# Attention and two gated MLPs on one core: the first pairs' transposes, sums and quotients move between the three banks

## The reference

```python
def phi(x):                      # x = q or k, scaled by D ** -0.25
    h = einsum('bhsd,md->bhsm', x, omega) - sum(x * x, -1) / 2
    return exp(h - max(h, -1)) / sqrt(m)
kv  = einsum('bhsm,bhsd->bhmd', k_p, v)
z   = sum(k_p, axis=2)
num = einsum('bhsm,bhmd->bhsd', q_p, kv)
den = einsum('bhsm,bhm->bhs', q_p, z) + 1e-06
x   = num / den                  # heads side by side: 2304 x 512
h = x @ w_in;  x = (h * clip(h + 3, 0, 6) / 6) @ w_out
h = x @ w_in2; x = (h * sigmoid(1.702 * h)) @ w_out2
```

## Time and profile before

| | us |
|---|---|
| median of 3 runs | 951.43 |
| lowest, highest | 950.95, 952.03 |
| the profiled execution | 951.39 |
| its span | 948.6 |
| TensorE busy (matmul) | 935.4 |
| VectorE, ScalarE, GpSimd busy | 398.7, 380.8, 170.1 |

### The profile page before, as it was taken

One profiled execution on the slowest core, in us unless ns is written; L12 is line 12 of the kernel. 1 busy time (PEld: TensorE's weight loads), 2 busy tenths in 40 slices (PEclk: granted clock), 3 DMA queues, 4 the chain that ended last, 5 costly groups with the idle time before them and its releaser, 6 DMA issues.

```text
span 948.6 us, 12977 instructions
## 1 busy us (share of the span) xinstructions
PE 935.4 (99%) x5126; PEld 784.9 (83%) x5126; DVE 398.7 (42%) x734; ACT 380.8 (40%) x871; POOL 170.1 (18%) x182
## 2 busy tenths in 40 slices
PE   8899999999999999999999999999999999999998
PEld 7778788878888788888889988888888888888898
DVE  6745665655446553452223442233224222422332
ACT  6656555554446544442225652232223222322322
POOL 2636466121212120000004830000000000000000
PEclk9999999999999999999999999999999999999999
DMA  8414342111121211010002610001001000100010
GB/s 275 153 50 151 118 139 63 52 50 34 55 63 38 63 26 38 1 45 1 1 0 82 178 53 1 1 1 45 0 1 45 1 1 0 45 1 1 4 41 24
DMA packets 40731, 45.99 MB, mean 48 GB/s; under 512 B 21600, under 2 KB 22240, under 8 KB 40672
## 3 DMA queue, kind: packets, MB, share of 16 engines
q1 hardware_dynamic: 40304, 44.54, 15.4%
q10 hardware_dynamic: 368, 0.62, 0.2%
HBM read 40.44 MB, written 4.72 MB: 48 GB/s over the span
## 4 chain that ended last, share of the span: by engine, by line
PE 96%; DVE 3%; ACT 0%; issue 0%; DVEq 0%
PE acc L604 14%; PE acc L606 14%; PE acc L605 14%; PE hid L581 11%; PE hid L585 10%; PE hid L582 10%; PE att L581 4%; PE att L585 4%; PE att L582 4%; PE att L509 3%; PE att L475 3%; PE att L549 2%; PE att L495 1%; DVE row_max L850 1%; PE att L468 1%; DVE h_max L865 0%
## 5 line engine op out<-in xcount | busy, mean ns | idle before, releaser
L604 PE MATMUL acc<-g_hi,w_out_hi 128*128 128x512 f32 (+1 forms) x640 | 241.5, 377 | 0.0
L606 PE MATMUL acc<-g_hi,w_out_lo 128*128 128x512 f32 (+1 forms) x640 | 236.1, 369 | 0.0
L605 PE MATMUL acc<-g_lo,w_out_hi 128*128 128x512 f32 (+1 forms) x640 | 235.9, 369 | 0.0
L581 PE MATMUL hid<-x_hi,w_in_hi 128*128 128x512 f32 (+1 forms) x476 | 181.6, 381 | 0.0
L585 PE MATMUL hid<-x_lo,w_in_hi 128*128 128x512 f32 (+1 forms) x476 | 176.0, 370 | 0.4 <-DVE x_lo L946 0.4
L582 PE MATMUL hid<-x_hi,w_in_lo 128*128 128x512 f32 (+1 forms) x476 | 175.4, 369 | 0.0
L961 DVE TENSOR_TENSOR g_lo<-R,g_hi 128x512 fp32r<-128x512 f32 (+1 forms) x160 | 110.8, 692 | 91.5 <-ACT g_hi L750 91.5
L604 PEld LDWEIGHTS acc<-g_hi,w_out_hi 128*128 128x128 f32 x640 | 120.7, 189 | 21.2 <-issue 1.9
L606 PEld LDWEIGHTS acc<-g_hi,w_out_lo 128*128 128x128 f32 x640 | 120.6, 188 | 20.5
L605 PEld LDWEIGHTS acc<-g_lo,w_out_hi 128*128 128x128 f32 x640 | 120.9, 189 | 19.6
L750 ACT ACTIVATE g_hi<-R 128x512 fp32r<-128x512 f32 (+1 forms) x160 | 94.6, 591 | 84.4 <-DVE R L956 52.6
(11 more groups left out here) (144 smaller groups left out, 1047.0 us busy)
## 6 DMA issues: line engine op xcount, KB each, us to landing
X<-w_in SPq DMA_DIRECT2D x16, 256.0 KB, 2.8
X<-w_out SPq DMA_DIRECT2D x16, 256.0 KB, 2.8
out_t<-X SPq DMA_DIRECT2D x16, 256.0 KB, 2.2
q_cols<-q_t SPq DMA_DIRECT2D x14, 288.0 KB, 2.9
k_cols<-k_t SPq DMA_DIRECT2D x14, 288.0 KB, 3.5
rows<-q_n SPq DMA_DIRECT2D x13, 288.0 KB, 3.6
rows<-k_n SPq DMA_DIRECT2D x13, 288.0 KB, 3.2
v_rows<-v_n SPq DMA_DIRECT2D x14, 256.0 KB, 3.2
```

What stands on the lines that cost most here:

```text
L581: nc.tensor.matmul(bank, w_hi[0][:, at], x_hi[:, k, x0:x0 + t], start=(k == 0), stop=False)
L604: nc.tensor.matmul(bank, w_hi[1][:, at], g_hi[:, g, 0:t], start=(s == 0), stop=False)
L605: nc.tensor.matmul(bank, w_hi[1][:, at], g_lo[:, g, 0:t], start=False, stop=False)
L606: last = nc.tensor.matmul(bank, w_lo[1][:, at], g_hi[:, g, 0:t], start=False, stop=(s == J - 1))
```

## The change

`three(a)` is turned the other way round for the pairs by token, with a new share of the uses:

- The query transposes of pair a+1, both heads, go into the bank of pair a's sums (`turn_bank`). The first head waits for `tails_out` (the sums are copied out) and the tail copies, the second for ScalarE's copy of the first.
- The sums of pair a+1 go into the second bank of pair a's quotient.
- The tail tile of pair a is turned back a pair later: by `key_values(a + 1)`, behind its sums in the same bank (`old_tails`). VectorE copies it out in `take_tails(a)`, placed behind the key statistics of a later pair.
- TensorE's order in the loop is now quotient(a), turn(a+1, 0), projection(a+2, "q"), turn(a+1, 1), projection(a+2, "k"), turn_back(a). ScalarE copies each transposed head right behind the key exponentials of the same head, and rounds `x_hi` behind the tails. VectorE takes the key statistics of pair 1 before the first sums.
- Behind pair 3, `turn(4, 0)` and `turn(4, 1)` come earlier, and the tail projection of pair 4 stands before the last two quarters of `hidden(0)`.

The diff (unchanged lines cut):

```diff
--- before.py
+++ after.py
@@ -208,7 +208,8 @@
         def three(a):
-            return tuple(att[(1 + min(a, LEAD - 1) + i) % 3] for i in range(3))
+            return tuple(att[(a - i) % 3 if by_token(a) else (2 + i) % 3] for i in range(3))
         def proj_banks(a, u):
@@ -218,18 +219,24 @@
...
         def turn_bank(a, h):
-            return three(a)[h]
+            if a == 0:
+                return three(0)[1 + h]
+            return three(a - 1)[0] if a < LEAD else three(a)[h]
         def kv_bank(a):
...
+        def old_tails(a):
+            return kv_bank(a)[:, P + 2 * (D + 1):2 * P + 2 * (D + 1)]
         def num_bank(a, h):
-            return three(a)[2 - h]
+            return three(a)[1 + h]
         def back_bank(a):
-            return three(a)[0]
+            return three(a)[1]
         def head_bank(a, half, h):
@@ -451,7 +458,7 @@
...
                 if a == LEAD - 1 and u == "tail":
-                    pe.wait_ge(x_ready, KC)
+                    pe.wait_ge(xs_ready, LEAD - 1)
                 elif a >= LEAD and u == "tail":
@@ -486,9 +493,11 @@
             def turn(a, h):
...
                 if 0 < a < LEAD and h == 0:
-                    pe.wait_ge(xs_ready, a)
+                    pe.wait_ge(tails_out, a)
+                    if a > 1:
+                        pe.wait_ge(x_written, 2 * (a - 1))
                 elif 0 < a < LEAD:
-                    pe.wait_ge(x_written, 2 * (a - 1) + 2)
+                    pe.wait_ge(turned_out, 2 * a + 1)
                 elif a >= LEAD:
@@ -498,9 +507,10 @@
             def key_values(a):
...
                 pe.wait_ge(exp_done, 5 * a + 5)
-                if by_token(a):
-                    pe.wait_ge(turned_out, 2 * a + 1)
                 nc.tensor.transpose(bank[:, 0:P], tile_of(a, KQ, 0, ST), ident[:])
+                if 0 < a < LEAD:
+                    pe.wait_ge(xs_ready, a)
+                    nc.tensor.transpose(old_tails(a), xs[:, ST, :], ident[:])
                 pe.wait_ge(load_v[in_set_b(a)], 48 * loads_in_set(a))
@@ -530,8 +540,8 @@
             def turn_back(a):
...
                 for t in range(ST):
-                    nc.tensor.transpose(back_bank(a)[:, t * P:(t + 1) * P], xs[:, t, :], ident[:])
-                nc.tensor.transpose(num_bank(a, 0)[:, 0:P], xs[:, ST, :], ident[:]).then_inc(xs_turned, 1)
+                    last = nc.tensor.transpose(back_bank(a)[:, t * P:(t + 1) * P], xs[:, t, :], ident[:])
+                last.then_inc(xs_turned, 1)
             def numerator(a, half):
@@ -542,6 +552,8 @@
...
                     pe.wait_ge(tails_out, a + 1)
+                    if a == LEAD - 1:
+                        pe.wait_ge(x_written, 2 * a)
                 tokens = slice(half * HALF, (half + 1) * HALF)
@@ -624,20 +636,20 @@
...
                 quotient(a)
+                turn(a + 1, 0)
                 projection(a + 2, "q")
-                turn(a + 1, 0)
+                turn(a + 1, 1)
+                projection(a + 2, "k")
                 turn_back(a)
-                projection(a + 2, "k")
-                turn(a + 1, 1)
             key_values(LEAD - 2)
...
             quotient(LEAD - 2)
+            turn(LEAD - 1, 0)
             hidden(0, (1,))
+            turn(LEAD - 1, 1)
             turn_back(LEAD - 2)
-            turn(LEAD - 1, 0)
-            turn(LEAD - 1, 1)
+            projection(LEAD - 1, "tail")
             hidden(0, (2, 3))
-            projection(LEAD - 1, "tail")
             for n in range(2 * L2):
@@ -779,20 +791,23 @@
...
                 square_rows(a, KK)
+            exps_of(1, "q")
             for a in range(LEAD - 2):
-                exps_of(a + 1, "q")
-                exps_of(a + 1, "k")
+                exps(a + 1, "k", 0)
+                turned_head(a + 1, 0)
+                exps(a + 1, "k", 1)
+                turned_head(a + 1, 1)
                 exps_of(a + 1, "tail")
-                turned_head(a + 1, 0)
                 first_high(a)
-                turned_head(a + 1, 1)
+                exps_of(a + 2, "q")
                 if a + 3 < LEAD:
...
                     square_rows(a + 3, KK)
-            exps_of(LEAD - 1, "q")
-            first_high(LEAD - 2)
+            exps(LEAD - 1, "k", 0)
             turned_head(LEAD - 1, 0)
             turned_head(LEAD - 1, 1)
+            first_high(LEAD - 2)
+            exps(LEAD - 1, "k", 1)
             for n in range(2 * L2):
@@ -818,7 +833,6 @@
...
                 if n == 0:
-                    exps_of(LEAD - 1, "k")
                     exps_of(LEAD - 1, "tail")
@@ -915,12 +929,15 @@
...
-            def take_back(a):
-                dve.wait_ge(xs_turned, a + 1)
+            def take_tails(a):
+                dve.wait_ge(kv_done, a + 2)
                 for h in range(2):
                     rows_h = slice(h * D, (h + 1) * D)
-                    nc.vector.tensor_copy(x_at(a, ST * P, TAIL, h * D, (h + 1) * D), num_bank(a, 0)[rows_h, rows_h]).then_inc(x_written, 1)
+                    nc.vector.tensor_copy(x_at(a, ST * P, TAIL, h * D, (h + 1) * D), old_tails(a + 1)[rows_h, rows_h]).then_inc(x_written, 1)
+            def first_low(a):
                 dve.wait_ge(x_hi_ready, a + 1)
@@ -937,6 +954,8 @@
...
                     keep(a)
+                    if a < LEAD:
+                        take_tails(a - 1)
             def split(c, blocks_k=range(KC), part=None):
@@ -985,20 +1004,26 @@
...
             maxima(1, "q")
+            maxima(1, "k")
             norms(1, KQ)
             biases(1, "q")
+            keep(0)
             norms(1, KK)
+            biases(1, "k")
             for a in range(LEAD - 2):
-                keep(a)
-                statistics(a + 1, "k")
+                if a > 0:
+                    keep(a)
+                    statistics(a + 1, "k")
+                    take_tails(a - 1)
                 statistics(a + 1, "tail")
...
                 statistics(a + 2, "q")
-                take_back(a)
+                first_low(a)
             keep(LEAD - 2)
+            take_tails(LEAD - 3)
+            statistics(LEAD - 1, "k")
             quotient(LEAD - 2)
-            take_back(LEAD - 2)
-            statistics(LEAD - 1, "k")
+            first_low(LEAD - 2)
             for n in range(2 * L2):
@@ -1007,7 +1032,7 @@
...
                     elif what == "kv":
-                        keep(a)
+                        attend(a, what)
                 for a, what in before:
```

## The result

The changed kernel takes 947.32 us (median of 6, 944.98 to 947.94), the one before 951.37 (median of 6): a ratio of 0.9954, 95% interval 0.9941 to 0.9966. That is 4.1 us faster, where 5.7 was forecast; 947.32 lies 1.6 above the forecast of 945.7. The profiled execution took 947.79, with a span of 944.9.

The account below looks back on a forecast made before the run. TensorE, busy 99% of the span, bounds the kernel, so only idle and low-clock time can be gained. Clock 1.7 plus idle 4.1 less 0.1 back gives 5.7 us: 951.4 to 945.7, own range 944.8 to 946.9, 8-in-10 range 943.7 to 947.8.

Parts of the forecast that it names:

- the idle time: TensorE, four stretches from 14.56 to 62.11: 7.04 us without a matmul, of which 4.1 are gained and 2.9 stay.
- Pair 0: First stretch: earlier transposes and turn-back bring sums(1) to 23.6 from 26.7; SP's queue, 1.1 later, stays hidden.
- The 1.1 us term: Pair 1, VectorE: the keys' small h_max stands behind GpSimd's fold addition until 29.09; 1.1 us lost, bounds 0 and 1.4.
- Pair 2: Query bias caught behind GpSimd's subtraction, key bias then not, or the reverse; about one stop, sums(3) at 43.2 or 44.05.
- Last pair: From sums(3) to the first output: 0.6 idle before turn(4,1), first output at 56.0 to 56.6, middle 56.3.
- 1.7 of clock: First stretch, mean grant 0.86 over 12.14 us: 1.7 us of lost full clock counted as gain.
- rival B: TensorE's low clock comes again; a fall costs about 1.7, giving 947.4; chance 0.14.
- signs named for being wrong: A fall of the clock, h_max at 0.2 throughout, a period over 10.5, or a new gap behind the first output.
- A: VectorE's small operations slip past GpSimd: periods of 9.1, first output near 54.4, time 943.8; chance 0.13.
- C: VectorE's order becomes the wait: a second stop a pair, 1.2 more in two pairs, 948.1; chance 0.08.
- D: Slower: one bank for both heads makes turn(a+1,1) wait for ScalarE's copy; stops at most 3.9 a pair, 955.5; chance 0.02.
- E: Nothing to measure: the waits only move behind the tail copies, 951; chance 0.03.

## Why the prediction was right or wrong

**What bounds the kernel, and the idle time.** Right. The 47.55 us of the kernel before, recorded with a fall, became 41.66 at full clock, 5.9 less, for 5.8 forecast. TensorE's time without a matmul fell from 7.04 to 2.6 (41.66 less 39.07), for 2.9 forecast, and its matmul time by 1.4.

**Pair 0.** Right: sums(1) at 23.48 for 23.6, SP's later queue hidden.

**Pair 1.** The 1.1 us term, bounded by 0 and 1.4, was right in place and size: h_max at 27.65, 1.33 long. That GpSimd's fold was the cause is shown by the kernel that moved the fold alone. The rule from the Trainium skill, SBUF — State Buffer, section "SBUF: two separate sides", agrees: 28.98 beside 28.95, none of the 1.39 shared.

**Pair 2.** Right at full clock (9.18 for 9.4): the query bias was caught and the key bias freed. With a fall it failed: "if the query bias is not caught, the key bias is" took them for alternatives, and in the profiled execution both were caught (1.01 and 1.33), as the sums came later against the rest.

**Last pair.** Right: 0.55 idle before turn(4,1) for 0.6, and the first output 12.95 to 13.26 after the sums for 13.1.

**The clock is the step that failed**, in two places. The term "1.7 of clock" took the longer matmul time of the stretch for time to be gained. In the kernel before, a fall costs 0.55 in time, 0.9 in pair 0: much of what the clock takes there, the wait for the copies would have taken. This left the sum unharmed, as that wait went too; it only stood under the wrong name. The other place did harm: rival B, "the low clock comes again", at 947.4 and a chance of 0.14, is what happened in six of 16 executions and in four of the first six. I argued that gaps of 1.4 and 1.2 had left the clock alone and mine were at most 1.1. But the grant fell in two records at the end of a gap of 1.07 and 1.08, and in another kernel it stayed up through gaps of 1.07 and 1.10, so the length doesn't tell. I also priced a fall at 1.7; it costs 2.3, as it brings the stop back in pair 2. Two of the signs named for being wrong came with it, the fall and a period over 10.5 (11.52). The Trainium skill, TensorE: Matmul & The Clock Gate, section "Part 1: The HAM clock gate", has the place of a transition variable from run to run. These executions agree and go further: of one program, eight of 16 were at 1.000 and six at 0.998, so even whether it falls varies.

**The sum** came out at 945.7, beside 945.5 at full clock, 945.9 as the median of all 16 executions and 947.3 as the median of the first six. It set a recorded execution with a fall against a timetable at full clock. That 947.32 lies so near B's 947.4 is in part luck: it is the middle of 946.85 and 947.79, and the executions with a fall have a mean of 947.8.

**Rivals.** A is not what the changed kernel does. The nearest to it is the version with the folds later and the squares first, where the key stop is gone and the query stop is covered: pair 1 takes 9.1, the first output starts at 54.58 for 54.4, and the time is 944.2 for 943.8. C's second stop a pair did come in pair 2 with a fall (1.01 and 1.33), but the query's part of it didn't reach TensorE, for VectorE waits 0.86 before keep (37.38). D's chain is short as it was said to be, but only by the order on ScalarE: with the copies behind it costs 3.7. That everything would only move (E) is out.

**Open.** What makes the clock fall, and where it fell in the kernel with the folds alone. Why two executions with dummies took 946.7 and 947.0 at full clock: they are 0.8 to 1.3 above the other three, about what the stop in pair 2 costs (1.08), but neither was recorded.

## What to carry to other kernels

When a reordering brings a tiny VectorE operation of two SBUF inputs on the path, look for what GpSimd does at that moment: its whole instruction can stand in front of it, and a semaphore wait that starts GpSimd a little later (here one line) is the cure. Count a stretch at the lower clock as lost time only up to the next wait that would have been there anyway, and look whether the delay lets two engines meet that passed each other before. And an engine's wait for a late operand is a free place for other work of that engine: the squares moved into it brought another 1.0 us (945.21 to 944.15), where the removal of the gap by itself had brought 0.4.

## What the runs showed of the hardware

- One program on one chip runs with and without a fall of TensorE's clock. Over all chips the grant was 0.998 in six of 16 executions of the changed kernel and in nineteen of 39 of the kernel before. In the three records with a fall the grant drops within 0.2 us of the end of a gap, of 1.07, 1.08 and 1.64 us. With six dummy matmuls in the gap none of ten executions fell; but with gaps of 1.07 and 1.10 left open in another order, only one of 11 did.
- A stop can catch the second of two dependent small operations alone (0.17, then 1.15) when GpSimd's next instruction starts in between, or both one after the other (0.89 and 0.52, the second behind a copy of 0.61).
